# An attention and two-layer kernel: v loaded beside k and q, products of ones ahead of the scores, and another order in the softmax and in the last quad

## The reference

```
qn = q / (norm(q, axis=1) + 1e-6);  kn likewise            # q, k, v: 6016 x 256
s  = kn.T @ qn / tau                                        # 256 x 256
a  = exp(s - max(s));  a /= a.sum(-1) + 1e-9
x  = v @ a                                                  # 6016 x 256
x  = (h - tanh(h)) @ w_out1,  h = x @ w_in1                 # w_in: 256 x 2048, w_out: 2048 x 256
out = elu(h) @ w_out2,        h = x @ w_in2
```

## Time and profile before

| what | value |
|---|---|
| median of 3 runs | 1035.82 us (1035.64 to 1036.03) |
| profiled execution, its own time | 1035.49 us |
| its span, first to last instruction | 1033.7 us |
| granted TensorE clock, mean over the span | 1.000 |
| TensorE busy | 99% of the span |
| VectorE, ScalarE busy | 79%, 74% |
| HBM read, written | 33.03 MB, 12.32 MB |

### The profile page before, as it was taken

How to read it: one execution, slowest core, us unless ns; L and a number is a source line. 1 busy time by engine, 2 the same in 40 slices (tenths; PEclk the granted TensorE clock), 3 DMA queues, 4 the chain that set the end, 5 groups by cost and what they waited for, 6 DMA issues and landing times.

```text
span 1033.7 us, 13703 instructions
## 1 busy us (share of the span) xinstructions
PE 1022.2 (99%) x4556; PEld 855.3 (83%) x4556; DVE 820.3 (79%) x1362; ACT 764.9 (74%) x1360; POOL 0.8 (0%) x7
## 2 busy tenths in 40 slices
PE   8999999999999999999999999999999999999997
PEld 7868888888888888888998888888888888888997
DVE  5889977867867776777998888887887887787775
ACT  6577776766666766767778878777778787778774
POOL 0000000000000000000000000000000000000000
PEclk9999999999999999999999999999999999999999
DMA  9932003003003001012212002102101201200202
GB/s 354 304 64 41 1 25 58 1 22 62 1 1 77 1 1 42 1 37 76 62 52 97 1 1 62 21 0 60 23 1 42 42 1 36 42 1 1 42 1 36
DMA packets 117558, 46.24 MB, mean 45 GB/s; under 512 B 100336, under 2 KB 108528, under 8 KB 117232
## 3 DMA queue, kind: packets, MB, share of 16 engines
q1 hardware_dynamic: 113344, 43.99, 16.1%
q10 hardware_dynamic: 4144, 1.38, 0.6%
HBM read 33.03 MB, written 12.32 MB: 44 GB/s over the span
## 4 chain that ended last, share of the span: by engine, by line
PE 98%; DVE 1%; DMA 1%; ACT 0%; issue 0%; DVEq 0%
PE r_ps L321 16%; PE r_ps L323 16%; PE r_ps L322 16%; PE x_ps L321 6%; PE x_ps L322 6%; PE x_ps L323 6%; PE z_ps L321 4%; PE z_ps L323 4%; PE z_ps L322 4%; PE x_ps L328 2%; PE y_ps L322 2%; PE q_ps L322 2%; PE y_ps L323 2%; PE q_ps L321 2%; PE q_ps L323 2%; PE y_ps L321 2%
## 5 line engine op out<-in xcount | busy, mean ns | idle before, releaser
L577 ACT ACTIVATE g_hi<-g 128x512 fp32r<-128x512 f32 (+1 forms) x384 | 236.5, 616 | 144.7 <-DVE g L804 58.4
L663 DVE TENSOR_TENSOR g_lo<-g,g_hi 128x512 fp32r<-128x512 f32 (+1 forms) x384 | 259.7, 676 | 50.3 <-ACT g_hi L577 41.5
L321 PE MATMUL r_ps<-g_hi,w_out_hi 128*128 128x512 f32 (+1 forms) x768 | 296.0, 385 | 0.0
L323 PE MATMUL r_ps<-g_hi,w_out_lo 128*128 128x512 f32 (+1 forms) x768 | 295.8, 385 | 0.0
L322 PE MATMUL r_ps<-g_lo,w_out_hi 128*128 128x512 f32 (+1 forms) x768 | 295.7, 385 | 0.0
L321 PEld LDWEIGHTS r_ps<-g_hi,w_out_hi 128*128 128x128 f32 x768 | 144.2, 188 | 27.4 <-issue 0.4
L323 PEld LDWEIGHTS r_ps<-g_hi,w_out_lo 128*128 128x128 f32 x768 | 144.2, 188 | 26.9
L322 PEld LDWEIGHTS r_ps<-g_lo,w_out_hi 128*128 128x128 f32 x768 | 144.2, 188 | 26.7
L321 PE MATMUL x_ps<-t_hi,w_ops 128*128 128x512 f32 (+1 forms) x288 | 111.5, 387 | 0.0
L322 PE MATMUL x_ps<-t_lo,w_ops 128*128 128x512 f32 (+1 forms) x288 | 111.0, 385 | 0.0
L323 PE MATMUL x_ps<-t_hi,w_ops 128*128 128x512 f32 (+1 forms) x288 | 110.9, 385 | 0.0
(11 more groups left out here) (107 smaller groups left out, 1478.1 us busy)
## 6 DMA issues: line engine op xcount, KB each, us to landing
v_blocks<-v_dram SPq DMA_DIRECT2D x40, 128.0 KB, 3.0
x_scratch<-side SPq DMA_DIRECT2D x20, 256.0 KB, 2.0
vt<-x_scratch SPq DMA_DIRECT2D x20, 256.0 KB, 3.5
out_dram<-v_blocks SPq DMA_DIRECT2D x80, 64.0 KB, 1.9
k_ring<-k_dram SPq DMA_DIRECT2D x9, 512.0 KB, 8.9
q_ring<-q_dram SPq DMA_DIRECT2D x9, 512.0 KB, 9.8
w_in_sb<-moe_w_in_dram SPq DMA_DIRECT2D x1, 2048.0 KB, 9.3
w_out_raw<-moe_w_out_dram SPq DMA_DIRECT2D x1, 2048.0 KB, 15.7
```

What stands on the lines that cost most here:

```text
L321: nc.tensor.matmul(ps, w_hi, m_hi, start=start, stop=False, skip_group_check=True)
L323: return nc.tensor.matmul(ps, w_lo, m_hi, start=False, stop=stop, skip_group_check=True)
L577: nc.scalar.activation(g_hi[b][n % DEPTH[b]][:, 0:width], g[b][:, 0:width], ACT.Copy).then_inc(g_rounded[b], 1)
L663: return nc.vector.tensor_tensor(lo, x, hi.bitcast(F32), ALU.subtract)
```

## The change

The constants, the loads of v, and products of ones ahead of the scores:

```diff
+PE_WARM = 9
-WF_ORDER = [(0, 0), (0, 1), (1, 0), (1, 1), (2, 0), (2, 1), (3, 0), (3, 1)]
+WF_ORDER = [(0, 0), (1, 0), (0, 1), (1, 1), (2, 0), (2, 1), (3, 0), (3, 1)]
+V_BESIDE = (6, 7, 8, 9)
...
-            def load_v(p):
+            def load_v(p, blocks=range(C // BLOCK)):
...
                 if i == RING:
                     sp.dma_start(tau_sb, tau.rearrange("(a b) -> a b", a=1).to_broadcast([P, 1])).then_inc(loaded_tau, 16)
-            load_v(0)
+                if i in V_BESIDE:
+                    x = 2 * V_BESIDE.index(i)
+                    load_v(0, (x, x + 1))
...
+            pe.wait_ge(ones_ready, 1)
+            for _ in range(PE_WARM):
+                nc.tensor.matmul(R[1][1][:, 0:P], ones[:, :], ones[:, :], start=True, stop=True, skip_group_check=True)
...
+                if i == LAST:
+                    transpose_prob(0)
                 last = scores(i, 1, range(CHUNKS[i]))
             last.then_inc(scores_ready, 1)
-            transpose_prob(0)
```

The last quad on TensorE:

```diff
             product(n, P1, X, True).then_inc(p1_done, 1)
-            pe.wait_ge(p5_copied, n)
-            product(n, P5, Q, True).then_inc(p5_done, 1)
             second(n - 1, "11")
             pe.wait_ge(y_seeded, n + 1)
             product(n, P6, X, False).then_inc(p6_done, 1)
-            product(n, P2, Y, False).then_inc(h_ready["11"], 1)
+            pe.wait_ge(p5_copied, n)
+            product(n, P5, Q, True).then_inc(p5_done, 1)
             pe.wait_ge(z_seeded, n + 1)
             product(n, P7, Z, False).then_inc(p7_done, 1)
             product(n, P3, X, False).then_inc(p3_done, 1)
+            product(n, P2, Y, False).then_inc(h_ready["11"], 1)
             second(n - 1, "22")
             second(n - 1, "12")
             pe.wait_ge(h_ready["22"], n + 1)
             product(n, P4, Z, False).then_inc(h_ready["21"], 1)
-            second(n - 1, "21")
             second(n, "22")
             second(n, "12")
+            second(n - 1, "21")
             second(n, "11")
             second(n, "21")
```

ScalarE, at the softmax and in the last quad (`lack` is the last step of `low` for "11" and "21", taken out so that other work can stand between the two):

```diff
+            round_t(0, P2)
             exp_scores(0)
+            round_t(0, P5)
             copy_aT(0)
             exp_scores(1)
-            round_t(0, P2)
-            round_t(0, P5)
+            round_t(0, P6)
             copy_aT(1)
             copy_wf(0)
-            round_t(0, P6)
+            round_t(0, P3)
             copy_wf(1)
-            round_t(0, P3)
-            copy_wf(2)
-            round_w(0)
-            copy_wf(3)
             round_t(0, P4)
             round_t(0, P7)
+            copy_wf(2)
+            copy_wf(3)
+            round_w(0)
...
+            n = ALL - 1
+            act.wait_ge(p1_done, n + 1)
+            act.wait_ge(g_ready["11"], n)
+            copy_bank(Y, X, n, y_seeded)
+            round_g(n - 1, "21")
+            act.wait_ge(p6_done, n + 1)
+            act.wait_ge(g_ready["21"], n)
+            copy_bank(Z, X, n, z_seeded)
+            act.wait_ge(p5_done, n + 1)
+            act.wait_ge(g_ready["12"], n)
+            copy_bank(h12, Q, n, p5_copied)
+            low(n, "22", h22)
+            low(n, "12", h12)
+            low(n, "11", Y)
+            round_g(n, "22")
+            lack(n, "11")
+            round_g(n, "12")
+            low(n, "21", Z)
+            lack(n, "21")
+            round_g(n, "11")
+            round_g(n, "21")
```

VectorE. `sum_w1` waits for 3, 4, 6 and 8 copies instead of 2, 4, 6 and 8. The steps of the softmax and of the last quad, in their new order:

```diff
             transpose_v(0, 0, 0)
+            transpose_v(0, 0, 1)
             dve.wait_ge(rooted, 1)
...
-            transpose_v(0, 0, 1)
+            transpose_v(0, 1, 0)
+            transpose_v(0, 1, 1)
             dve.wait_ge(rq_ready, 1)
...
+            scale_scores(0)
+            form_t(0, P5)
             split_t(0, P1)
+            invert_sum(0)
             split_t(0, P2)
+            scale_scores(1)
             split_t(0, P5)
             form_t(0, P6)
+            invert_sum(1)
             split_t(0, P6)
-            sum_w1(0)
-            split_t(0, P3)
             form_t(0, P4)
             form_t(0, P7)
-            split_w(0)
+            split_t(0, P3)
             split_t(0, P4)
             split_t(0, P7)
+            sum_w1(0)
+            split_w(0)
...
+            n = ALL - 1
+            add_rows_of_quad(n)
+            elu_low(n, "22")
+            form_g(n, "22", h22)
+            elu_low(n, "12")
+            form_g(n, "12", h12)
+            split_g(n, "22")
+            form_g(n, "11", Y)
+            split_g(n, "12")
+            form_g(n, "21", Z)
+            turn_last(0, 1)
+            split_g(n, "11")
+            turn_last(1, 1)
+            split_g(n, "21")
+            turn_last(0, 0)
+            turn_last(1, 0)
```

More of the change, by code:

```diff
@@ L219, in _ @@
             q_rows = q[0].rearrange("(p r) c -> p r c", p=P)
-            def load_v(p):
+            def load_v(p, blocks=range(C // BLOCK)):
                 n = 2 * WIDTH[p]
                 rows = v[0, TOKEN0[p]:TOKEN0[p] + n, :].rearrange("(e i) c -> i e c", i=BLOCK)
[L224 to L228, removed]
+                for block in blocks:
+                    cc, b = divmod(block, P // BLOCK)
+                    channel = block * BLOCK
+                    sp.dma_start(v_blocks[b * BLOCK:(b + 1) * BLOCK, cc, 0:n].rearrange("i (e c) -> i e c", c=BLOCK),
+                                 rows[:, :, channel:channel + BLOCK]).then_inc(loaded_v, 16)
             for i, rows in enumerate(CHUNKS):
@@ L341, in _ @@
                 if i == LAST:
-                    pe.wait_ge(ones_ready, 1)
                     pe.wait_ge(summed, SUMMED_ALL)
@@ L569, in low, with lack @@
                     nc.scalar.activation(g[b][:, 0:width], src[:, 0:width], ACT.Exp).then_inc(low_step[b], 1)
-                    act.wait_ge(low_step[b], n - FIRST2 + 1)
-                    nc.scalar.activation(g[b][:, 0:width], g[b][:, 0:width], ACT.Relu, bias=1.0, scale=-1.0).then_inc(low_ready[b], 1)
+                    if n < ALL - 1:
+                        lack(n, b)
+            def lack(n, b):
+                width = place(n)[2]
+                act.wait_ge(low_step[b], n - FIRST2 + 1)
+                nc.scalar.activation(g[b][:, 0:width], g[b][:, 0:width], ACT.Relu, bias=1.0, scale=-1.0).then_inc(low_ready[b], 1)
             def round_g(n, b):
@@ L590, in move_rows @@
                 nc.scalar.activation(side[:, m, j, 0:width], R[m][j][:, 0:width], ACT.Copy).then_inc(r_moved[j], 1)
-            for n in range(ALL):
+            for n in range(ALL - 1):
                 p, u, width, part = place(n)
@@ L619, in _ @@
                 low(n, "11", Y)
-                if n == ALL - 1:
-                    break
                 if n == 0:
@@ L725, in sum_w1 @@
             def sum_w1(i):
-                dve.wait_ge(wf_copied, 2 * (i + 1))
+                dve.wait_ge(wf_copied, (3, 4, 6, 8)[i])
                 sum_w(2 * i, 2)
@@ L768, in _, with scale_scores @@
             norm_step(nc.vector.tensor_scalar(rk, inv_norm[:, CC:2 * CC], inv_tau[:, 0:1], None, ALU.mult))
-            transpose_v(0, 0, 1)
+            transpose_v(0, 1, 0)
+            transpose_v(0, 1, 1)
             dve.wait_ge(rq_ready, 1)
[L771 to L774, removed]
+            def scale_scores(m):
                 dve.wait_ge(scores_ready, m + 1)
@@ L779, in _, with invert_sum @@
                 nc.vector.tensor_reduce(neg_max[:, m:m + 1], prob[:, m, :], AX.X, ALU.max, negate=True).then_inc(max_ready, 1)
-            form_t(0, P5)
-            for m in range(CC):
+            def invert_sum(m):
                 dve.wait_ge(exp_ready, m + 1)
@@ L904, in _, with turn_last @@
                 split_g(n, "22")
[L905 to L922, removed]
+            def turn_last(m, j):
+                if m == 0:
+                    dve.wait_ge(r_ready[j], 2 * PAIRS)
+                else:
+                    dve.wait_ge(g_used[("21", "12")[j]], ALL)
+                turn_out(PAIRS - 1, m, j, R[m][j])
+            n = ALL - 1
[14 more added lines that the diff above has]
+            turn_last(1, 0)
 INPUTS = ["q", "k", "v", "tau", "moe_w_in", "moe_w_out", "moe2_w_in", "moe2_w_out"]
```

## The result

The changed kernel took 1042.55 us (median of 6 runs, 1041.22 to 1043.22) against 1036.12 (1035.64 to 1036.48) for the kernel before on the same chip: ratio 1.0061, 95% interval 1.0048 to 1.0074. Forecast was 1037.5, with a range up to 1040.0. The sign of the likeliest case was right; the size was not.

The account below looks back on a forecast made before the run. The prediction took TensorE, 98% of the chain, as the bound, with DMA engines about full until v is in. Head +2.9 (3.9 + 0.2 - 1.2) and tail -1.2 on 1035.49 gave 1037.2, plus 0.33 for the median 1037.5; range 1034.0 to 1040.0.

Parts of the forecast that it names:

- the likeliest case: Whole kernel: a later head outweighs an earlier tail, so slower, at 1037.5 us; chance 0.55.
- The sums of squares follow the landing: Ahead of the norms: the last sum comes 3.3 us after the last q, so norms at 45.4, +3.9 us.
- v beside: Loads at the start: v queued ahead of the last k and q makes the last q land 5.7 us later.
- That SyncE is held is no cost by itself: Load queue: holding SyncE costs nothing, since two v loads and a chunk always stay queued; no size added.
- Rival D: Load queue: three of four v pairs let it run dry 1 us each, norms 3 us later, 1040.5; chance 0.05.
- rival B: Scores behind the norms: the clock falls while TensorE waits for sums, costing 1.8 us, total 1039.3; chance 0.22.
- The point of 4.5: TensorE's wait ahead of the norms: the clock falls from about 4.5 us of idleness on; 4.3 us was expected.
- Warm products: Ahead of the scores: nine products of ones take 3.9 us and save 1.8, lost entirely in the wait for sums.
- Transposes and softmax: Head behind the scores: early transposes cost +0.2 us; second scaling to first quad product shrinks from 12.1 to 10.9, -1.2.
- what is late next is w_ops: End of the softmax stretch: w_ops sets the first quad product at 10.9 us; TensorE is ready at 10.3.
- the two ahead of the root end with it: VectorE before the square root: two v transposes are covered; without that cover they would cost 0.1 us.
- The last quad: End of the kernel: half the stores leave before the last transposes, the last land in 1.9 us, -1.2 us.

Follow-up runs that it names:

- c3: The changed kernel with the four pairs of v loads behind chunks 10 to 13 instead of 6 to 9; 1040.65 us.
- a3: The changed kernel with v loads one each behind chunks 6 to 13 instead of two each behind 6 to 9; 1042.88 us.
- c2: The changed kernel with the first tiles' v loads issued from GpSimd's queue instead of SyncE's; 1040.47 us.
- a2: The changed kernel with 18 more products of ones where TensorE waits for the last sums; 1040.51 us.
- b2: The kernel before with only the nine products of ones added ahead of the scores; 1036.14 us.
- a1: The changed kernel with the eight v loads put back behind chunk 13, everything else kept; 1034.53 us.
- b1: The kernel before with only the v loads moved behind chunks 6 to 9; 1044.42 us.
- b3: The kernel before with only the new order of softmax and fused weights and the early transposes; 1035.03 us.
- b4: The kernel before with only the new order of the last quad; 1035.86 us.
- c1: The changed kernel with v loads back behind chunk 13, v's transposes behind the root's steps, and P2's rounding behind the first exponential; 1034.12 us.
- c4: As c1, with half of w_in1 loaded ahead of v, v's transposes behind both scalings, and ScalarE and VectorE work reordered; 1036.23 us.

## Why the prediction was wrong

**The step that failed** is "The sums of squares follow the landing", with its 3.3 us from the last q. I took VectorE's lag behind the last landing for a constant. It was what was left of a backlog at chunk 11: 6.86 us of squares and additions that follow each other once q 11 is in. In the kernel after, the lag behind q 13 was 4.2 us. The right question was which landing the chain of sums waits for last. Before, the answer stood on ScalarE (32.75, `<-DMA`, against 36.60, `<-DVE`). By it and the landing delay that was measured the last sum ends at 39.6 + 7.3 = 46.9 and the norms start at 47.0, as they did. Twelve of the thirteen profiles have 6.85 to 6.93 us from the landing of q 11 to the last sum, while the lag behind q 13 goes from 2.7 to 4.2 in them; the 3.3 that I read in one profile was no constant. c3 is the thirteenth, in which the other limit decides.

This step makes 1.6 us of the miss. Leaving the clock out of the likeliest case makes 1.9, the tail 0.7, the softmax -0.15, together 4.0 in the profiled execution; its median lies 1.3 us above it where I had added 0.3. So even with the right landing the forecast would have been 1039.1.

**v beside, a term mis-sized.** Forecast +5.7 at the last q, measured +6.4, inside the bounds; at q 11, with all eight loads ahead of it in both, +7.3. That is 0.91 us a load against 0.71 in the forecast and 0.82 by its upper bound. It is no constant of the chip. Against the mean of the profiles with v behind (33.3) the delay of q 11 is 6.7 us with eight loads ahead of it, 0.84 a load; 5.9 with five (a3), 1.2 a load; 3.6 with two (c3), 1.8 a load. Why fewer cost more each is open; in c3 part of it is the dry queue. Full DMA engines at 159 GB/s were the right row; the difference of two landings (36.3 and 42.0) was too small a measure, since a v load was already under way beside the last q. "That SyncE is held is no cost by itself" fits c2, where the delay is nearly the same without long holds, but not c3, where the queue ran dry behind one. Rival D in its stated form (the queue dry for 1 us in three of the four pairs) didn't occur in the kernel after.

The section "Why small descriptors are slow" of the Trainium skill's "DMA: Bandwidth & Descriptors", by whose three beats a packet I had estimated 4.4 us, speaks in the right direction; the delay measured is larger, 6.7 to 7.3 us.

**The clock.** I gave rival B 0.22 and set its point at 4.5 us of idleness. The wait was 4.04, shorter than that, and the clock was at 0.5 from 48.21 to 51.62: the scores behind the norms cost 1.8 us, as B had priced them. a2 shows the cause, and a price of 1.7 us by the profiles. The point of 4.5 was read from two rows, 4.84 us at the start that were enough and 4.4 at the end that were not. That the second sets a lower bound for every other place was my guess; waits of 1.3 (b2) and 1.9 us (a1) were followed by a fall too.

In b1 and a3 6.8 us ran at 0.5. The profiled execution of the kernel after has a mean clock of 0.998; of its other runs one has 0.997 and those at 1042.5 us and above 0.996. 3.4 us at half rate are 0.0016 of the mean of a span of 1039 us, so the slower ones fit two such stretches, which would cost 3 to 4 us in place of 1.8. This is inference, as only one of the six was profiled. It would explain why the median lies 1.3 us above the profiled execution, and why c2, with 0.998 in every run, is 2 us faster with norms only 0.4 us sooner.

**Warm products.** They took 3.61 us from 0.99, forecast 3.9 from 0.95, and the first scores ran at 0.216. That the gain would be lost in the wait for the sums was right. In the kernel before alone (b2) the result was the same.

**Transposes and softmax.** Forecast -1.2 from the second scaling to the first product, measured -1.36. The split of w_ops ends at 67.08 and TensorE, 10.7 us after the scaling instead of the 10.3 I gave it, comes at 67.24: it ends the stretch itself, and "what is late next is w_ops" is off by 0.2 us. b3 alone gave 1.1 (its interval includes no change). a1 shows what I passed over: "the two ahead of the root end with it" holds only while v is in. When v lands at 42.95 they hold up the root by 1.9 us. Since the change loads v early this cost nothing in it.

**The last quad, a term mis-sized.** Forecast -1.2, measured -0.5. The last store was issued when it was before, as said (1036.54 against 1030.21, 0.07 later after the head's 6.26 is taken off). But it took 2.5 us to land, not 1.9: the last eight stores still queue behind each other, and 1.8 is the time of the first of eight alone. TensorE's last records came 0.5 us later, forecast 0.25: waits of 0.25 and 0.17 for the copies to Y and Z, and second products with records 0.207 apart where they had been 0.203. This did reach the stores. Before, each queue issued its eight in one row from 1026.47 on and never waited for the last transposes. After, ScalarE's queue had been idle since 1033.36 and issued its last four from 1035.03, right behind the first of the last two transposes (1034.35 + 0.65), so the last issue now hangs on TensorE's end. By these rows 0.25 us less of delay would have put it about 0.2 us ahead of its old place (an estimate). b4 shows the same 0.5 us in its profile and 0.25 in its medians, which is inside its interval.

Sum in the profiled execution: sums +5.5 at the norms (forecast 3.9), transposes and the clock +2.1 to the second scaling (0.2), softmax -1.36 (-1.2): head +6.3 (2.9), tail -0.5 (-1.2), together +5.75 in the span.

## What to carry to other kernels

When a load is moved ahead of others, don't shift the end of what depends on them by the delay of the last landing: find the instruction that last waited for a DMA before its engine ran without a gap, shift that one, and check it against the last landing plus the work that must follow it. Loads in small pieces cost the queue more than their bytes, and ahead of the critical loads they delay all of these. And a wait that an engine enters because it was made faster can cost the clock as well; some products of ones in it gave back about 2 us.

## What the runs showed of the hardware

- **Short waits and the clock.** A wait of 4.0 us ahead of the norms went with a fall in all four profiles that have it; in two the clock fell behind the wait (after, b1), in two 2.8 and 3.1 us into it (c3, a3). With products in it there was none (a2). Of shorter ones, 1.3 (b2), 1.9 (a1) and 2.3 us (c2, ahead of the norms) were followed by a fall; 1.7 us (c1, at 49.3), 1.9 (c2, at 21.3) and 2.05 (c4, at 61.4) were not. What decides between these is open. The slow stretch was 3.4 us long in some executions (after, a1, b2, c2) and 6.8 in others (b1, a3, c3).
- **An issue can be held by what is queued ahead.** A load of 128 KB in pieces of 128 B let the next issue on SyncE wait 2.5 to 6.5 us, and one at a time (a3) was no better than two. From GpSimd's queue such loads took 0.78 us of issuing each, and SyncE's own issues, which then ran far ahead of the landings, were held for 2.04 us at most.
- **A hold can leave the queue dry**: a share of 0.26 and 50 GB/s from 30 to 32 us in c3.
- **v's price at q 11**: 0.84 to 0.91 us for a load of 128 KB with eight ahead of it (144 to 156 GB/s, where k and q move at 422), more for each with fewer ahead.
- **Landings scatter**: with the same loads in the same order ahead of it, q 11 landed from 32.7 to 34.2 us in seven profiles, so 0.4 us between two single profiles says nothing.
